# Products of the identity on TensorE in front of the answers and low scores of pairs 1 to 3

## The reference, cut to what matters

```
for t in range(S):                                   # S = 768, D = 40, 4 x 8 heads
    y[:, :, t] = einsum('bhd,bhde->bhe', r_t, state)
    Sa = einsum('bhde,bhe->bhd', state, a_t)
    state = state * w_t - outer(Sa, b_t) + outer(v_t, k_t)
h = x @ w_in;  g = h - tanh(h);  x = g @ w_out       # x: 3072 x 320, F = 2048
for e in range(4):                                   # F = 1024
    out += p[:, e:e+1] * (relu(x @ w1[e]) @ w2[e])
```

## Time and profile before

| what | value |
|---|---|
| median of 3 runs | 1577.67 us (1575.66 to 1582.25) |
| profiled execution, its own time | 1579.84 us |
| span of the profiled execution | 1578.1 us |
| TensorE busy (products) | 1467.6 us, 93% of the span |
| VectorE, ScalarE, GpSimd busy | 822.9, 403.7, 367.6 us |
| mean granted clock of TensorE | 0.975 of full |

### The profile page before, as it was taken

One profiled execution on the slowest core, in us unless ns is written; L12 is line 12 of the kernel. 1 busy time (PEld: TensorE's weight loads), 2 busy tenths in 40 slices (PEclk: granted clock), 3 DMA queues, 4 the chain that ended last, 5 costly groups with the idle time before them and its releaser, 6 DMA issues.

```text
span 1578.1 us, 37807 instructions
## 1 busy us (share of the span) xinstructions
PE 1467.6 (93%) x15888; PEld 1280.9 (81%) x15888; DVE 822.9 (52%) x1448; ACT 403.7 (26%) x824; POOL 367.6 (23%) x313
## 2 busy tenths in 40 slices
PE   3388889999999999999969999999999999999998
PEld 3366678778878978977958988999999999999997
DVE  8868678788778786943213333333333333333333
ACT  1132433333333333333323221111111111111111
POOL 6111545243333331311325202020010202020000
PEclk9967799999999999999989999999999999999999
DMA  7354782174165064030030311001010101000011
GB/s 193 80 142 127 190 216 81 56 189 105 37 171 141 1 174 105 1 89 20 1 108 1 104 54 37 0 0 37 0 37 0 37 0 37 0 0 0 0 50 50
DMA packets 85708, 105.29 MB, mean 67 GB/s; under 512 B 13331, under 2 KB 65555, under 8 KB 85579
## 3 DMA queue, kind: packets, MB, share of 16 engines
q1 hardware_dynamic: 84226, 102.75, 24.3%
q10 hardware_dynamic: 1352, 0.66, 0.2%
HBM read 74.24 MB, written 29.13 MB: 66 GB/s over the span
## 4 chain that ended last, share of the span: by engine, by line
PE 81%; DVE 11%; issue 2%; ACT 2%; DMA 1%; POOL 1%; SPq 1%; POOLq 1%; DVEq 0%; ACTq 0%
PE banks L1609 22%; PE banks L1619 21%; PE banks L895 10%; PE banks L904 9%; DVE tmp L1162 2%; PE banks L659 2%; DVE ld L1159 2%; PE banks L777 2%; DVE nvmak L1219 2%; PE banks L739 2%; PE banks L752 2%; PE banks L722 1%; PE banks L731 1%; PE banks L781 1%; PE banks L632 1%
## 5 line engine op out<-in xcount | busy, mean ns | idle before, releaser
L1609 PE MATMUL banks<-x2t,u 128*128 (+1 forms) x1536 | 376.7, 392 | 0.0
L1619 PE MATMUL banks<-u,hid 128*128 128x320 f32 x2304 | 362.5, 309 | 0.0
L1619 PEld LDWEIGHTS banks<-u,hid 128*128 128x128 f32 x2304 | 349.8, 188 | 13.1 <-issue 0.9
L1713 DVE SCALAR_TENSOR_TENSOR hid<-banks,hid 128x512 fp32r<-128x512 f32 x192 | 132.9, 692 | 404.4 <-ACT hid L1699 404.4
L1609 PEld LDWEIGHTS banks<-x2t,u 128*128 128x128 f32 x1536 | 282.5, 188 | 52.6
L1699 ACT ACTIVATE hid<-banks 128x512 fp32r<-128x512 f32 x192 | 114.7, 597 | 564.9 <-PE banks L1609 564.9
L895 PE MATMUL banks<-xt,wi 128*128 128x512 f32 x768 | 195.7, 399 | 14.6 <-POOL xt L1396 13.6
L904 PE MATMUL banks<-wo,hid 128*128 128x320 f32 x1152 | 183.5, 310 | 2.0 <-POOL hid L1401 1.6
L904 PEld LDWEIGHTS banks<-wo,hid 128*128 128x128 f32 x1152 | 174.5, 188 | 10.8 <-POOL hid L1401 3.9
L895 PEld LDWEIGHTS banks<-xt,wi 128*128 128x128 f32 x768 | 141.3, 190 | 43.3 <-POOL xt L1396 13.9
L1401 POOL TENSOR_TENSOR hid<-shared,hid 128x512 fp32r<-128x512 f32 x96 | 124.4, 1296 | 210.9 <-ACT hid L1074 210.9
(11 more groups left out here) (129 smaller groups left out, 1526.9 us busy)
## 6 DMA issues: line engine op xcount, KB each, us to landing
scaled_operands<-made SPq DMA_DIRECT2D x76, 192.4 KB, 3.8
kb<-scaled_operands SPq DMA_DIRECT2D x44, 192.0 KB, 3.6
made<-kbaw SPq DMA_DIRECT2D x38, 192.0 KB
made<-kbaw SPq DMA_DIRECT2D x41, 144.0 KB
raw<-w SPq DMA_DIRECT2D x8, 640.0 KB, 5.7
lam<-scaled_operands SPq DMA_DIRECT2D x44, 96.8 KB, 3.1
at<-scaled_operands SPq DMA_DIRECT2D x44, 96.0 KB, 3.0
raw<-w SPq DMA_DIRECT2D x8, 512.0 KB, 4.0
```

Of the source, the lines that this page charges most:

```text
L1609: mm = pe.matmul(self.p_up[f][:], self.u1[:, par, w, f * 128:(f + 1) * 128], self.xt[:, bass.ds(n, 1), x, :].rearrange("p o t -> p (o t)") ...
L1619: mm = pe.matmul(self.p_dn[t][:, 0:D], self.hid[:, f, h, t * 128:(t + 1) * 128], self.u2[:, par, w, f, :], start=(f == 0 and i == 0), stop ...
L1713: dve.scalar_tensor_tensor(out=ex.hid[:, f, 1, :], in0=ex.p_up[f][:], scalar=0.0, in1=ex.hid[:, f, 0, :].bitcast(F32), op0=ALU.max, op1=AL ...
```

## The change

A new function `keep_clock(p, n)` makes n float32 products of the 128 x 128 identity with itself into columns 256 to 383 of `answer_bank`, which nobody reads. It does so for p = 1, 2 and 3 only, without waiting for anything and without raising a counter. It is called before the answers of block 0 (8 products), before those of blocks 1, 2 and 3 (4 each) and before the low scores of the next pair (3): 23 products in each of three pairs, 69 in all.

```diff
+        def keep_clock(p, n):
+
+            if 0 < p < PPC:
+                for _ in range(n):
+                    pe.matmul(answer_bank[:, 2 * C:3 * C], ident[:], ident[:], start=True, stop=True)
+
...
             if p and not after_mlp:
                 scores_ur(p - 1)
+            keep_clock(p, 8)
             answer(p, 0, 0)
             answer(p, 1, 0)
             right_sides(p, 0, 1)
...
             if p > 2:
                 state_by_values(p)
+            keep_clock(p, 4)
             answer(p, 0, 1)
             answer(p, 1, 1)
...
             if more:
                 scores(p + 1, 0)
+            keep_clock(p, 4)
             answer(p, 0, 2)
             answer(p, 1, 2)
             result_by_keys(p)
...
             if p <= 2:
                 state_by_values(p)
+            keep_clock(p, 4)
             answer(p, 0, 3)
             answer(p, 1, 3)
...
             if more:
                 natural(p + 1, 1)
+                keep_clock(p, 3)
                 scores_low(p + 1)
             turn_answers(p)
```

## The result

The changed kernel takes 1584.63 us (median of 11 runs, 1580.99 to 1590.66), the kernel before 1577.67 (11 runs): ratio 1.0048, 95% interval 1.0037 to 1.0059. That is 7 us more, just inside the 0.5% bound, which the interval reaches over; forecast were 2.2 more. The profiled execution took 1587.44 us with a span of 1585.7, so it is one of the longer ones.

What follows compares the result with a forecast made beforehand. Bound in pairs 1 to 3: TensorE's chain at half clock until about 120 us, then VectorE's steps. Terms 0.7 + 1.2 + 0.3 = +2.2 us on 1577.67 gave 1579.9 us; range 1573 to 1588.

Steps and rivals of the forecast that it cites:

- the likeliest case: Whole kernel: the forecast itself, a change of 0 to +6 us, most likely 1579.9 us; chance 56%.
- The price of a product: On TensorE: 0.27 us at full clock from L722, 0.51 at 0.5 from L739; bounds 0.16 and 0.65.
- Pair 1, predicted +0.7: Products' cost in pair 1: +3.9 at the last answers, then -2.0 and -0.7 for work no longer at 0.5, 0.5 lost.
- Pair 2, predicted +1.2: Products' cost in pair 2: clock falls again at its start, later groups mostly covered; together with pair 1 +1.9.
- L752, the eight, the work to the end of L649: Pair 2's start: L752 saves 0.9, the eight cost 3.9, the work to L649 saves 1.0; +2.0 us.
- from there to L777: Pair 2, after the first four: work to L777 at full clock instead of 0.5; -1.7 us.
- The three lie under the wait before L792: 0: End of pair 2: the three products before the low scores are covered by TensorE's wait; 0 us.
- Pair 3, predicted +0.3: Pair 3: VectorE sets the pace, its waits cover most products; a few tenths left, above all of the last four.
- The clock is held, or the products are cheap: Rival for pairs 1 and 2: clock up at pair 2's start, 1578.2 us, or 1576.5 with 0.16 a product; chance 27%.
- Products that don't raise the clock: Rival for pairs 1 to 3: identity products don't count as work; sum 21 us, 1599 us, slower; chance 7%.
- The case of a dearer product or pauses: Rival: 0.65 us a product costs 12 more, 1592 us, or TensorE pauses, 0.3 in proportion; chance 7%.
- Faster by over 0.5%: Rival: cold work on TensorE's chain in pairs 1 and 2 gives back 9.0 us, over the 7.9 bound; chance 3%.

Runs made afterwards that it cites:

- the five profiles: Profiles of programs without products in pairs 1 to 3, three of them of the kernel before; their mean for pair 1 is 24.4 us.
- the run with covered products: Against the kernel before: 8, 4, 4 and 3 products in pair 3 and 3 in pair 2, only under TensorE waits; 1575.05 us, ratio 0.9990.
- the fours and threes alone: The change without the eights: 4, 4, 4 and 3 products in each of pairs 1 to 3; 1580.38 us, ratio 1.0024 against the kernel before.
- 276 harmless instructions: Kernel before plus 69 tiny 32 x 32 x 32 products under pair 0's wait, none of the change's products; 1578.84 us, ratio 1.0018.
- the padded change: The change plus 17 tiny products under pair 0's wait, displacing the program by 344 instructions; 1581.12 us, ratio 1.0036 against the kernel before.
- the padded kernel before: Kernel before plus 22 tiny products (88 instructions) under pair 0's wait, no product elsewhere; 1573.56 us, ratio 0.9992.
- the last two kernels: Products ahead of the wait, three before low scores: five in pairs 1 to 3, padded, 1570.93 us; six in pairs 1 and 2, unpadded, 1571.32 us.
- the doubled products: The change with every group doubled (16, 8, 8, 8, 6) and 12 tiny products in pair 0; 1592.23 us, ratio 1.0103 against the kernel before.
- the five ahead of the wait: Against the kernel before: five products ahead of the wait, three before low scores, pairs 1 to 3, 62 tiny products; 1570.93 us, ratio 0.9964.

## Why the prediction was right, and where its sizes were off

The forecast was no change beyond 0.5% with +2.2 us; measured are +7, 1584.63 us, inside the range of 1573 to 1588 and within 0.5%, near its edge. It lies outside the 0 to +6 us of the likeliest case. That it stayed within 0.5% is in part luck: pair 2 cost three times what was forecast, and displacement wasn't in the sum.

*The price of a product.* Predicted 0.27 at full clock and 0.51 at 0.5. The changed kernel shows 16 instructions in 2.05 us, of which the last alone is 0.27: 0.119 from one to the next, or 0.24 a product, about 0.25 with the groups of four (1.16 us for 8 instructions). At 0.5, 8 in 2.08 us and 0.55 for the last: 0.44. At full clock the price from L722's pairs was right within a tenth or so, at 0.5 it was 0.07 too high; loads ran beside products, as the earlier trace rows said. The prediction's upper bound of 0.65 did not occur at full clock, nor did the 0.43 that it had estimated from the rule on overlap (the Trainium skill, TensorE: Matmul & The Clock Gate, "What overlaps and what doesn't").

*Pair 1, predicted +0.7.* The terms were added up wrongly: +3.9 at the last answers, -2.0, a loss of 0.5 and -0.7 make +1.7, and the loss was subtracted. The sum should have read +3.2, the forecast 1580.9. Against the first profile the single steps held: the eight in 3.57 us (3.7 predicted), the clock up behind them, the first answers 3.2 later, the next 2.9 (2.7 + 0.7 predicted), the scores behind them 1.25 (1.7). As a whole, pair 1 came out 1.8 us shorter than in the first profile. The pauses make that: from L722 to the result by state (L731, now L737) it is 4.43 us before and 1.99 after.

```profile
94.18 1.09 PE L722 MATMUL banks<-nvmak,kbn 128*64 128x128 f32 x16
...
98.61 1.22 PE L731 MATMUL banks<-rt,sn 104*64 104x128 f32 x16
```

```profile
96.52 1.09 PE L728 MATMUL banks<-nvmak,kbn 128*64 128x128 f32 x16
...
98.51 1.09 PE L737 MATMUL banks<-rt,sn 104*64 104x128 f32 x16
```

Without these 2.4 us pair 1 costs +0.6. Against the mean of the five profiles it is +0.3. But the -2.0 and -0.7 for work at 0.5 from 99.43 on are a saving only where the pause at 97 us had pulled the clock down. Against the four profiles without it (mean 22.7) the products cost 2.0.

*Pair 2, predicted +1.2, measured +3.2 in the means and +3.9 in the first two profiles: the step that failed.* The first profiles of the two kernels, both counted from the end of pair 1's low scores, show where:

| step of pair 2 | predicted | measured |
|---|---|---|
| L752, the eight, the work to the end of L649 | +2.0 | +3.2 |
| four before the answers of block 1 | +0.7 | +0.7 |
| from there to L777 | -1.7 | -1.6 |
| third four, read at VectorE's next right side (L1184) | 0 | +0.3 |
| fourth four, read at VectorE's mask (L1219) | +0.2 | +0.8 |
| three before the low scores | 0 | +0.4 |

The clock fell as L752's successor began, not behind it, so its saving of 0.9 didn't come (2.08 us again; in the second profile of the change it did come, 1.16, and the pair took 23.48), and the work to L649 won 0.5 instead of 1.0, against eight products that cost 3.7 instead of 3.9. The last three rows come from one mistake. The sentences "The third four lie in time that VectorE's steps fill: 0", "The fourth delay the scores a little: +0.2" and "The three lie under the wait before L792: 0" took the cover of the first profile as given. It was there only because TensorE had been on time; now VectorE waits 0.38 and 0.72 us for TensorE. Its mask then ends 1.3 us behind the scores (L781) instead of 2.1, which no longer covers the three products. With nothing ahead to delay TensorE they are covered (21.12 us in the run with covered products). The -1.7 came against this profile, but it is a saving only where there is a stretch at 0.5 until 119.91.

*Pair 3, predicted +0.3, measured +1.0 in the means, +1.7 in the first two profiles.* That VectorE covers 8, 4 and 4 is shown by the run with covered products (26.90 us with and without). The last four were said to cost "a few tenths"; they ran at 0.5 (2.08 us) and VectorE waited 1.73 behind them, and the three behind cost 0.4 as in pair 2. In the other two profiles of the change the last four took 1.16 and 1.25 us and the pair 27.66 and 27.63, still 0.7 over 26.90. With the fours and threes alone it took 26.90, so their price hangs on the clock and on what stands ahead.

*The sum* is thus 4.5 us by the profiles and 4.7 to 7 by the medians for the products, where the terms gave 2.2.

*What the sum didn't have*: displacement. I had put pauses at 0.3 us in proportion to the added instructions. What counts isn't their number but where the rest of the program comes to lie: +2.8 us for 276 harmless instructions (interval 0.6 to 5.0), -1.3 for 88 (not told from 0). In the profiles the stretch between pairs 7 and 22 is 6.0 and 2.5 us longer in the change than in the first profile of the kernel before, and as long as there (483.7 against 483.8) once the change is padded. By the medians, some 2 (the padded change) to 2.8 of the 7 us are this, and both figures have an error of that size.

*The rivals.* "The clock is held, or the products are cheap" did not come in the time (1578.2 or less), though the clock was held in pair 1 of one profile of the change. Products that don't raise the clock are out: 1599 was far off, and the clock was at 0.5 for 17 us instead of 44. The case of a dearer product or pauses was half right: the product was not dearer, but pauses between 300 and 700 us had been put at 0.3. "Faster by over 0.5%" didn't happen for this placement, but its premise did, in another place: products under the wait ahead of the fall go with a gain of 0.4 to 0.5% (0.3% against the padded kernel before). The advice against idle gaps between bursts that the prediction weighed (the Trainium skill, the same page, "Why this matters for your kernels") points the way of these two runs, which fill the gap itself; the changed kernel filled the time behind it. TensorE's waits in question have 1.0 to 1.6 us here.

What stays open: what makes the pauses, whether they alone pull the clock down near 99 us, and why the profiled executions of the last two kernels lie so high among their runs. How much of the 0.4 to 0.5% won comes from each pair, and how much from displacement, was not tried. Nor is it known why the clock stayed up near 85 us in the second profile of the change, with nothing ahead of the wait.

## What to carry to other kernels

Filler work that is to hold TensorE's clock belongs ahead of a wait, no longer than the wait, as in the two fastest runs here. Behind the wait it stands on the path: in most profiles it ran at the low clock there, and the three pairs together came out longer. Idle time that would cover it must be looked for anew once something ahead has moved, since an engine that was early may now be late. A saving from low clock must be read from several profiles, since its stretches move from one execution to the next. And where instructions are added to a long program (276 to 37807 here), a kernel with as many harmless ones should be measured before a difference of 0.2% is put down to their work.

## What the runs showed of the hardware that was not expected

TensorE pauses 0.5 to 3.3 us for nothing that the profile shows, at the same instructions in two kernels of equal displacement (0.93 and 1.00, 1.46 and 1.18, 1.19 and 1.19 us), and elsewhere with other displacements. The padded change and the covered products have no pause of 0.5 us; the padded kernel before, the doubled products and the five ahead of the wait, padded in the same way, have them (1.15, up to 0.76, up to 1.88 us). The length changes between executions of one kernel: the pause near 97 us of the kernel before was 1.29, 1.43 and none in three profiles. The queue of program loads has 101 loads with 1.65 MB before and 102 with the 276 instructions added, so a piece of program that arrives late is a possible cause; this is argued, and no run varied these loads by themselves.

A product of 128 x 128 x 128 in float32 takes 0.24 to 0.25 us at full clock, although each of its two instructions loads weights for 0.19 us.
